# One core's attention and experts kernel: the first expert's last 640 tokens in Strassen's form, the attention blocks packed closer

## The chip, the core and the metric

One core of one Trainium2 chip. The metric is device time in microseconds (us), of the whole program. TensorE is PE in the profile, VectorE DVE, ScalarE ACT, GpSimd POOL, SyncE SP; L757 is line 757 of the kernel before.

## The reference

All in fp32: attention in a band, then four experts, then one layer with a rational function.

```
scores = q k^T / 8, masked to a band (4 plain heads: the last 32 keys; 4 dilated: every 4th of 128)
x   = softmax(scores) v                    -> 1152 tokens x 512
for e in 0..3: x2 += p[:, e] * (relu(x @ w1[e]) @ w2[e])       w1 512x1024, w2 1024x512
h   = x2 @ w_in;  g = P(h) / (Q(h) + 1e-6);  out = g @ w_out   w_in 512x2048
```

## The kernel before

**Precision.** Every operand of TensorE is split in a high and a low part (fp32r): ScalarE copies the high part, VectorE or GpSimd subtracts for the low one, and each product is three matmuls: hi hi, hi lo, lo hi.

**Iterations.** `ITER` lists (expert, first token, tokens). Expert 0 has four, of 256, 256, 256 and 384 tokens; experts 1 to 3 have two each, of 640 and 512; then six of 384 for the rational layer, which is kept as two more experts. An iteration has 8 chunks (`FC`) of 128 hidden columns. Slot (k, f): `inner_product(k, f)` makes a chunk of h (4 x 3 matmuls, L673), ScalarE takes relu of it (`high`), VectorE the low part (`low`), and `outer_product` of the chunk `LAG` = 3 slots before adds h w2 into the sums of each tile of 128 tokens (3 matmuls of 512 columns for each tile, L757). `take_sums` (VectorE) keeps the sums.

**Strassen's form** (in Winograd's variant, L731) is used by experts 1 to 3: chunks go in 4 pairs, each pair in 7 products of half the tokens and half the depth (6 matmuls each) in place of 8. It needs sums of weight quarters S1 to S4 (`sum_pair` on GpSimd, `high_pair` on ScalarE, `low_pair` on GpSimd) and of token quarters T1 to T4 (`transform` on VectorE, `high_t` on ScalarE, `low_t` on VectorE), and `combine` on VectorE makes the quarters C of the result by way of U2 and U3. `snapshot` (ScalarE) copies "A11 B11" out before "A12 B21" is added to it. The T parts of tokens 0 to 640 and 640 to 1152 are made beside the 384-token iteration of expert 0 and serve all three experts.

**Attention** comes in 20 blocks of two heads: 16 big ones (256 tokens: units 0 to 3 times 4 head pairs) and 4 small ones (the 128 tokens that remain). A block w goes: `scores(w)` on TensorE; `mask`, `maximum` on VectorE; `exponentials` on ScalarE (4 of big, 2 of small); `invert` on VectorE; `normalise` on GpSimd; `turn(w)` on TensorE; `take_turned` on ScalarE; `values(w)` on TensorE; `attention_hi` on ScalarE, `attention_lo` on VectorE. In a slot with block w TensorE does inner product, `turn(w)`, outer product, `values(w)`, `scores(w + 2)`, and the helpers do the softmax of w + 1. Blocks 0 to 5 come in a part written out by hand ahead of slot (0, 4). `block_of_slot` puts blocks 6 to 19 in every second slot of iterations 0 and 1, in slot (1, 7), and in slots 0 to 6 of iteration 2; the 384-token iteration has none.

**Order.** Each engine runs one written list, and waits only by semaphores; nothing overtakes. GpSimd's list holds `normalise(w)`, the low parts of expert 0's weights (`low_w1`, `low_w2`) and the mask of the small dilated blocks (`make_rest_mask`, a string of selects). SyncE issues all loads in one list (`load_qk`, `load_v`, `load_inner`, `load_outer`, `load_raw1`); a load waits until its buffer is read.

```
            normalise(9)
            make_rest_mask()
            for w in range(10, BLOCKS):
                normalise(w)
```

## Time and profile before

| | us |
|---|---|
| runs | 641.30, 641.62, 642.65: median 641.62 |
| profiled execution | 640.78, its span 639.0 |
| TensorE busy | 631.6 |
| VectorE, ScalarE, GpSimd busy | 389.6, 318.0, 269.1 |
| L757 outer products, chain's share | 46% |
| L673 plain inner products, chain's share | 23% |
| L731 Strassen products, chain's share | 20% |

The span is the time from the first instruction to the last. Matmuls overlap, so a matmul's own duration is longer than its distance to the next; the chain of waits shows the distance. The granted clock of TensorE is full in all 40 slices of the span.

### The profile page before, as it was taken

How to read it: one execution, taken by the hardware profiler on the slowest of the kernel's cores; microseconds unless marked ns; L12 is line 12 of the kernel's file. 1: busy time of each engine (PE TensorE's matmuls, PEld its weight loads, DVE VectorE, ACT ScalarE, POOL GpSimd, SP SyncE). 2: the span in 40 equal slices, each digit the busy share in tenths (PEclk: the TensorE clock that was granted, in tenths of full speed). 3: DMA queues.
4: the chain of work that ended last, by engine and by line, in shares of the span. 5: the costliest groups of instructions: out<-in, count | busy, mean ns of one | idle time of the engine just before them, and what ended most of it. 6: DMA issues, size and time to landing. Idle time of an engine off the chain costs nothing.

```text
span 639.0 us, 10664 instructions
## 1 busy us (share of the span) xinstructions
PE 631.6 (99%) x4008; PEld 561.5 (88%) x4008; DVE 389.6 (61%) x760; ACT 318.0 (50%) x740; POOL 269.1 (42%) x283
## 2 busy tenths in 40 slices
PE   8999999999999999999999999999999999999998
PEld 6888888898888898898899898889998999889996
DVE  6534543937755445325456325438988788889896
ACT  6864552335322333212343212346887777877774
POOL 6763112049830794301784101145712576732221
PEclk9999999999999999999999999999999999999999
DMA  8942210002220131000122100101530000001011
GB/s 289 292 157 87 72 34 1 2 33 73 94 66 2 67 100 66 34 2 2 66 100 67 34 0 2 67 34 52 186 126 1 1 1 1 2 0 50 2 49 51
DMA packets 21684, 37.68 MB, mean 59 GB/s; under 512 B 3520, under 2 KB 4160, under 8 KB 21632
## 3 DMA queue, kind: packets, MB, share of 16 engines
q1 hardware_dynamic: 21632, 36.99, 17.5%
q8 instruction: 32, 0.52, 0.3%
q14 instruction: 20, 0.16, 0.1%
HBM read 34.62 MB, written 2.36 MB: 58 GB/s over the span
## 4 chain that ended last, share of the span: by engine, by line
PE 93%; SPq 2%; DVE 2%; ACT 1%; DMA 1%; issue 1%; POOL 0%; DVEq 0%; ACTq 0%
PE banks L757 46%; PE banks L673 23%; PE banks L731 20%; PE banks L645 1%; PE banks L616 1%; PE banks L626 1%; DMA scratch<-in_qk_dil 1%; ACT scratch L881 1%; SPq L562 1%; PE banks L793 1%; PE banks L633 0%; SPq L507 0%; DVE h_lo L1300 0%; DVE acc L1206 0%; DVE acc L1201 0%
## 5 line engine op out<-in xcount | busy, mean ns | idle before, releaser
L757 PE MATMUL banks<-w_hi,h_hi 128*128 128x512 f32 x432 | 171.7, 397 | 0.1
L757 PE MATMUL banks<-w_lo,h_hi 128*128 128x512 f32 x432 | 170.6, 395 | 0.0
L757 PE MATMUL banks<-w_hi,h_lo 128*128 128x512 f32 x429 | 169.9, 396 | 0.0
L1520 POOL TENSOR_TENSOR w_lo<-raw,w_hi 128x512 fp32r<-128x512 f32 x32 | 41.2, 1310 | 157.8 <-ACT w_hi L934 157.8
L673 PE MATMUL banks<-x_hi,w_hi 128*128 128x384 f32 (+1 forms) x320 | 104.9, 328 | 0.0
L673 PE MATMUL banks<-x_lo,w_hi 128*128 128x384 f32 (+1 forms) x320 | 102.5, 320 | 0.0
L673 PE MATMUL banks<-x_hi,w_lo 128*128 128x384 f32 (+1 forms) x320 | 102.3, 320 | 0.0
L1293 DVE TENSOR_TENSOR stage<-banks,stage 128x320 f32<-128x320 f32 (+1 forms) x120 | 54.1, 455 | 78.1 <-PE banks L731 74.9
L757 PEld LDWEIGHTS banks<-w_hi,h_lo 128*128 128x128 f32 x429 | 80.5, 188 | 19.3
L757 PEld LDWEIGHTS banks<-w_lo,h_hi 128*128 128x128 f32 x432 | 81.2, 188 | 14.5
L757 PEld LDWEIGHTS banks<-w_hi,h_hi 128*128 128x128 f32 x432 | 81.2, 188 | 14.6 <-issue 0.4
L1534 POOL TENSOR_TENSOR h_lo<-rational,h_hi 128x384 fp32r<-128x384 f32 x47 | 47.7, 1015 | 108.6 <-ACT h_hi L1092 108.6
L979 ACT ACTIVATE h_hi<-stage 128x320 fp32r<-128x320 f32 (+1 forms) x72 | 31.4, 443 | 79.6 <-DVE stage L1293 79.4
L1300 DVE SCALAR_TENSOR_TENSOR h_lo<-stage,h_hi 128x320 fp32r<-128x320 f32 (+1 forms) x72 | 54.6, 768 | 24.6 <-ACT h_hi L979 23.2
L1493 POOL TENSOR_TENSOR w_lo<-raw,w_hi 128x512 fp32r<-128x512 f32 x40 | 53.8, 1359 | 28.9 <-ACT w_hi L917 28.3
L673 PEld LDWEIGHTS banks<-x_hi,w_hi 128*128 128x128 f32 x320 | 60.2, 188 | 4.6 <-DVE rational L1391 0.2
L673 PEld LDWEIGHTS banks<-x_lo,w_hi 128*128 128x128 f32 x320 | 60.3, 188 | 2.4
L673 PEld LDWEIGHTS banks<-x_hi,w_lo 128*128 128x128 f32 x320 | 60.3, 188 | 0.0
L1066 ACT ACTIVATE banks<-banks,b_sb 128x384 f32<-128x384 f32 x48 | 26.7, 556 | 36.4 <-PE banks L673 36.3
L1386 DVE SCALAR_TENSOR_TENSOR rational<-rational,b_abs,banks 128x384 f32<-128x384 f32 x48 | 29.4, 613 | 23.5 <-ACT rational L1067 23.2
L962 ACT ACTIVATE stage<-banks 128x320 f32<-128x320 f32 (+1 forms) x24 | 9.9, 410 | 58.0 <-PE banks L731 57.8
L1467 POOL TENSOR_TENSOR scratch<-scratch 128x384 f32<-128x384 f32 (+1 forms) x20 | 15.4, 772 | 50.3 <-DVE scratch L1164 50.2
(119 smaller groups left out, 1238.0 us busy)
## 6 DMA issues: line engine op xcount, KB each, us to landing
raw<-in_weights SPq DMA_DIRECT2D x48, 256.0 KB, 2.9
raw<-in_weights SPq DMA_DIRECT2D x16, 512.0 KB, 3.6
raw_last<-in_weights SPq DMA_DIRECT2D x16, 256.0 KB, 5.9
scratch<-in_v SPq DMA_DIRECT2D x16, 192.0 KB, 4.9
scratch<-in_qk_dil SPq DMA_DIRECT2D x8, 320.0 KB, 5.5
out_t<-acc SPq DMA_DIRECT2D x9, 256.0 KB, 2.1
scratch<-in_qk_plain SPq DMA_DIRECT2D x8, 272.0 KB, 4.4
scratch<-in_qk_rest SPq DMA_DIRECT2D x2, 256.0 KB, 2.8
```

Source lines behind the costliest of these rows:

```text
L673: last = nc.tensor.matmul(h_of(k, f), w[:, f, dc, :], x, start=dc == 0 and i == 0, stop=dc == DC - 1 and i == 2)
L731: last = nc.tensor.matmul(product_bank(name)[:, 0:n], w[:, d], x[:, d], start=opens and d == 0 and i == 0, stop=d == HALF - 1 and i == 2, ...
L757: last = nc.tensor.matmul(sum_bank(k, t), h[:, cols], w[:, f, :], start=f == 0 and i == 0, stop=f == FC - 1 and i == 2)
L979: nc.scalar.activation(quarter(k, p, name)[0], source, ACT.Relu).then_inc(quarter_hi, 1)
L1066: nc.scalar.activation(ps_q[:, 0:WIDE], h_of(k, f), ACT.Abs, scale=b_sb[:, 0:1])
L1293: nc.vector.tensor_tensor(out, bank, to, ALU.add).then_inc(combined, 1)
L1300: nc.vector.scalar_tensor_tensor(out=lo, in0=source[:, 0:n], scalar=0.0, in1=hi.bitcast(F32), op0=ALU.max, op1=ALU.subtract).then_inc(quar ...
L1386: nc.vector.scalar_tensor_tensor(out=qq[:, i], in0=sq[:, i], scalar=b1_abs[:, 0:1], in1=ps_q[:, 0:WIDE], op0=ALU.mult, op1=ALU.add).then_i ...
L1467: nc.gpsimd.tensor_tensor(p, p, row_inv[:, w % SOFT, 0:n].unsqueeze(2).to_broadcast([P, n, TK]), ALU.mult).then_inc(normed, 1)
L1493: nc.gpsimd.tensor_tensor(w2_lo[:, c], raw_of(e, c)[1], w2_hi[:, c].bitcast(F32), ALU.subtract)\
L1520: last = nc.gpsimd.tensor_tensor(w1_lo[:, 2 * p + c].rearrange("p a b -> p (a b)"), raw1[:, c], w1_hi[:, 2 * p + c].rearrange("p a b -> p ...
L1534: nc.gpsimd.tensor_tensor(h3_lo[:, c % RING, :], h_full[:, c % SLOTS], h3_hi[:, c % RING, :].bitcast(F32), ALU.subtract)\
```

## The change

- Expert 0 has three iterations: two of 256 tokens (tokens 640 to 896 and 896 to 1152) and, as iteration `KW` = 2, one of 640 tokens (0 to 640) in Strassen's form. Units are laid in token order so that units 0 and 1 are the first two iterations (`UNIT_AT`).
- Blocks 8 to 19 are reordered (`SEQUENCE`), head pairs 0 and 2 first. `VISITS` gives every slot from (0, 3) to (1, 6) a block, and (1, 1) and (1, 6) two. TensorE's turn(6) follows scores(7) with no product between. Outer products of a slot with two blocks go one tile to each block.
- T parts of tokens 0 to 640 are made beside slots (1, 2) to (1, 5) and (1, 7), those of the rest beside iteration 3. ScalarE copies them behind each slot's block steps.
- S parts of expert 0 are made by GpSimd between the normalises, and high_pair by ScalarE in slots (1, 2), (1, 4), (1, 7) and the first pair of iteration 2. Expert 0's raw weight pairs are loaded once more (`load_raw1(0, p)`).
- GpSimd's `make_rest_mask` moves behind normalise(10), low_w2(5) ahead of it. ScalarE's copies of expert 0's weights spread over more slots.
- The first Strassen pair has its own order of products, with two outer products between the first ones.
- On-chip memory is laid out anew (offsets only), and load order follows the blocks.

The diff, cut to what matters here; SyncE's list first, then TensorE, ScalarE, VectorE, GpSimd:

```diff
 FILLERS = (6, 2, 3, 2, 1)
-MASK_AT = (0, PAIRS // 2, BIG_BLOCKS)
+SEQUENCE = [(u, p) for u in (0, 1) for p in range(PAIRS)]
+SEQUENCE += [(u, p) for d in (0, 1) for u in range(2, UNITS + 1) for p in (d, d + PAIRS // 2)]
+VISITS = {(0, 3): (6,), (0, 4): (7,), (0, 5): (8,), (0, 6): (9,), (0, 7): (10,),
+          (1, 0): (11,), (1, 1): (12, 13), (1, 2): (14,), (1, 3): (15,), (1, 4): (16,), (1, 5): (17,), (1, 6): (18, 19)}
+MASK_AT = (0, PAIRS // 2, SEQUENCE.index((UNITS, 0)))
...
 WIDE = 3 * P
-ITER = [(0, 0, 2 * P), (0, 2 * P, 2 * P), (0, 4 * P, 2 * P), (0, 6 * P, WIDE)]
+ITER = [(0, 5 * P, 2 * P), (0, 7 * P, 2 * P), (0, 0, 5 * P)]
...
+KW = START[1] - 1
+PLAIN_CHUNKS = KW * FC
+UNIT_AT = (5 * P, 7 * P, 0, 2 * P, 4 * P)
...
-W1_HIGH_AT = ((4,), (), (5, 6), (), (7,), (), (), ())
-W2_HIGH_AT = ((0, 1), (), (2,), (), (3,), (4,), (5,), (6, 7))
+W1_HIGH_AT = ((4,), (), (5,), (6,), (7,), (), (), ())
+W2_HIGH_AT = ((0,), (), (1,), (2,), (3,), (4,), (5,), (6, 7))
...
-T_STEPS = (((0, 0, 0), (0, 0, 1)), ((0, 1, 0),), ((0, 1, 1),), ((1, 0, 0), (1, 0, 1)), ((1, 1, 0),), ((1, 1, 1),), (), ())
+T_STEPS = {2: ((0, 0),), 3: ((0, 1),), 4: ((0, 2),), 5: ((0, 3),), FC - 1: ((1, 0), (1, 1), (1, 2))}
+T_STEPS_MIDDLE = {2: ((0, 3),), 3: ((1, 2),)}
+T_STEPS_END = {0: ((0, 0),), 1: ((0, 1), (0, 2)), 2: ((1, 0), (1, 1)), 3: ((1, 3),)}
+T_OF_STEP = (("T1",), ("T3", "T2"), ("T4",), ())
+S_HIGH_AT = {2: 0, 4: 1, FC - 1: 2}
...
+            load_v(10)
+            load_qk(12)
+            for w in range(11, 15):
+                load_v(w)
+                load_qk(w + 2)
+            load_raw1(0, 0)
+            for w in range(15, 18):
+                load_v(w)
+                load_qk(w + 2)
+            load_v(18)
+            load_raw1(0, 1)
+            load_v(19)
             sp.dma_start(a_sb[:, :], a.partition_broadcast(P)).then_inc(ab_in, 16)
             sp.dma_start(b_sb[:, :], b.partition_broadcast(P)).then_inc(ab_in, 16)
-            for w in range(2 * PAIRS, 3 * PAIRS):
-                load_qk(w)
-                load_v(w)
+            load_raw1(0, 2)
+            load_raw1(0, 3)
             load_raw1(1, 0)
             for c in (0, 1):
                 load_raw2(1, c)
-            for w in range(3 * PAIRS, BLOCKS):
...
-                    w = block_of_slot(k, f)
-                    inner_product(k, f)
-                    if w is not None:
+                    ws = visits(k, f)
+                    if (k, f) != (0, LAG):
+                        inner_product(k, f)
+                    if not ws:
+                        outer_of_slot(k, f)
+                    for i, w in enumerate(ws):
                         turn(w)
-                    outer_of_slot(k, f)
-                    if w is not None:
+                        outer_of_slot(k, f, range(i, i + 1) if len(ws) > 1 else None)
                         values(w)
                         if w + 2 < BLOCKS:
                             scores(w + 2)
-            for f in range(FC):
-                inner_product(UNITS - 1, f)
-                outer_of_slot(UNITS - 1, f)
-            outer_product(UNITS - 1, FC - LAG)
-            for k in range(START[1], START[MOE]):
+            outer_product(KW - 1, FC - LAG)
+            winograd_product(KW, 0, "A11 B11")
+            outer_of_pair(KW, 0, 0)
+            winograd_product(KW, 0, "A12 B21")
+            outer_of_pair(KW, 0, 1)
+            for name in FIRST_PRODUCTS[2:]:
+                winograd_product(KW, 0, name)
+            for k in range(KW, START[MOE]):
                 for p in range(FP):
...
-                        continue
-                    high(k, f)
-                    if w is not None:
-                        take_turned(w)
-                        if k == 0 and f < LAG:
-                            high(k, f + 1)
-                        if w + 1 < BLOCKS:
-                            exponentials(w + 1)
-                        attention_hi(w)
+                    if (k, f) == (0, 2):
+                        high(0, 2)
+                        take_turned(5)
+                        high(0, 3)
+                        exponentials(6)
+                        attention_hi(5)
+                    elif k or f > LAG:
+                        high(k, f)
+                    for w in visits(k, f):
+                        steps_of_block(w)
                     if k == 0:
                         for c in W1_HIGH_AT[f]:
                             high_w1(c)
                         for c in W2_HIGH_AT[f]:
                             high_w2(0, c)
+                    else:
+                        for d, step in T_STEPS.get(f, ()):
+                            high_t_of_step(0, d, step)
+                        if f in S_HIGH_AT:
+                            high_pair(0, S_HIGH_AT[f])
             act.wait_ge(ab_in, 32)
             nc.scalar.activation(b1_abs[:, :], b_sb[:, 1:2], ACT.Abs).then_inc(b1_ready, 1)
-            for f in range(FC):
-                high(UNITS - 1, f)
-                for g, d, half in T_STEPS[f]:
-                    for t in ("T4",) if half else ("T1", "T3", "T2"):
-                        if (g, t) != (1, "T1"):
...
+                if step == 0:
+                    dve.wait_ge(xa_lo, BLOCKS if g or d else BLOCKS - PAIRS - 2)
...
-                    if w is not None and w + 1 < BLOCKS:
-                        mask(w + 1)
-                    if w is not None and w > PAIRS:
+                    ws = visits(k, f)
+                    for i, w in enumerate(ws):
+                        if w + 1 < BLOCKS:
+                            mask(w + 1)
                         attention_lo(w - 1)
-                    if w is not None and w + 1 < BLOCKS:
-                        maximum(w + 1)
-                    low(k, f)
-                    if k == 1 and f == 0:
+                        if w + 1 < BLOCKS:
+                            maximum(w + 1)
+                        if i == 0 and (k, f) != (0, LAG):
+                            low(k, f)
+                        if w + 1 < BLOCKS:
+                            invert(w + 1)
+                    if not ws:
+                        attention_lo(BLOCKS - 1)
+                        low(k, f)
+                    if (k, f) == (1, 0):
                         normalise_probs()
-                    if k == 0 and f < LAG:
-                        low(k, f + 1)
-                    if w is not None and w + 1 < BLOCKS:
-                        invert(w + 1)
                     if k and f == LAG - 1:
                         take_sums(k - 1)
-                    if w == BLOCKS - 1:
-                        attention_lo(w)
-            for f in range(FC):
-                if f == LAG - 1:
-                    take_sums(UNITS - 2)
-                low(UNITS - 1, f)
-                for g, d, half in T_STEPS[f]:
-                    transform(g, d, half)
-            for k in range(START[1], START[MOE]):
+                    if k:
+                        for d, step in T_STEPS.get(f, ()):
+                            transform(0, d, step)
+            transform(0, 1, 3)
+            for k in range(KW, START[MOE]):
...
             normalise(6)
             low_w1(0, 5)
+            low_w2(0, 1)
+            normalise(7)
+            low_w1(0, 6)
             low_w2(0, 2)
-            low_w1(0, 6)
-            normalise(7)
+            normalise(8)
+            low_w1(0, 7)
             low_w2(0, 3)
-            low_w1(0, 7)
+            normalise(9)
             low_w2(0, 4)
-            normalise(8)
             low_w2(0, 5)
+            normalise(10)
+            make_rest_mask()
             low_w2(0, 6)
+            normalise(11)
             low_w2(0, 7)
             nc.gpsimd.memset(log_bias[:, :], ONE_EPS * 2.0 ** -LOG_SHIFT)
             nc.gpsimd.memset(exp_bias[:, :], -LOG_SHIFT * math.log(2.0))
-            normalise(9)
-            make_rest_mask()
-            for w in range(10, BLOCKS):
-                normalise(w)
+            normalise(12)
+            normalise(13)
+            sum_pair(0, 0)
+            normalise(14)
+            normalise(15)
+            low_pair(0, 0)
+            normalise(16)
+            sum_pair(0, 1)
+            normalise(17)
+            low_pair(0, 1)
+            normalise(18)
+            normalise(19)
+            for p in (2, 3):
+                sum_pair(0, p)
+                low_pair(0, p)
```

## Rows read from the trace of the kernel before

**Rows 1.** The page, part 1: engine, busy us (share of span), instructions.
```profile
PE 631.6 (99%) x4008; PEld 561.5 (88%) x4008; DVE 389.6 (61%) x760; ACT 318.0 (50%) x740; POOL 269.1 (42%) x283
```

**Rows 2.** Waits of PE: who waited for whom: us in total, times, longest.
```profile
PE banks L731 <- DVE stage L1293: 0.9, 1, 0.9
```

**Rows 3.** The chain, 0 to 260 us: start us, us, what.
```profile
35.29 1.43 PE banks L673 x12
...
69.21 1.62 PE banks L673 x12
70.83 0.44 PE banks L626 x4
71.27 1.40 PE banks L757 x6
72.67 0.61 PE banks L645 x16
73.28 0.49 PE banks L616 x16
...
82.42 0.33 PE banks L616 x16
...
88.78 0.22 PE banks L626 x2
...
105.76 2.09 PE banks L673 x12
...
164.38 4.40 PE banks L731 x30
```

**Rows 4.** PE in order of time, about 26 us: start us, us, engine, line, what.
```profile
25.52 0.56 PE L616 MATMUL banks<-scratch 64*64 64x96 f32 x16
```

**Rows 5.** ACT in order of time, 70 to 135 us.
```profile
71.31 0.59 ACT L891 ACTIVATE scratch<-banks 96x512 f32<-96x512 f32 x1
...
73.33 0.63 ACT L895 ACTIVATE x_hi<-banks 128x256 fp32r<-128x256 f32 x1
...
133.33 0.83 ACT L937 ACTIVATE s_hi<-s_stage 128x768 fp32r<-128x768 f32 x1
```

**Rows 6.** POOL in order of time, 26 to 140 us.
```profile
27.24 0.83 POOL L1467 TENSOR_TENSOR scratch<-scratch 128x384 f32<-128x384 f32 x1
...
43.55 1.28 POOL L1493 TENSOR_TENSOR w_lo<-raw,w_hi 128x512 fp32r<-128x512 f32 x1
...
47.92 1.02 POOL L1436 TENSOR_SCALAR_AFFINE_SELECT scratch<-scratch 32x96 f32<-32x96 f32 x3
49.20 4.84 POOL L1436 TENSOR_SCALAR_AFFINE_SELECT scratch<-scratch 32x48 f32<-32x48 f32 x13 [0.26 <-POOL scratch L1436]
...
73.81 0.83 POOL L1467 TENSOR_TENSOR scratch<-scratch 128x384 f32<-128x384 f32 x1 [3.74 <-DVE scratch L1164]
...
86.62 0.51 POOL L1467 TENSOR_TENSOR scratch<-scratch 128x192 f32<-128x192 f32 x1 [2.85 <-DVE scratch L1164]
...
105.86 0.73 POOL L1513 TENSOR_TENSOR raw<-raw 128x256 f32<-128x256 f32 x1
...
135.50 1.85 POOL L1526 TENSOR_TENSOR s_lo<-s_stage,s_hi 128x768 fp32r<-128x768 f32 x1
```

**Rows 7.** DVE in order of time, 86 to 115 us.
```profile
86.46 1.39 DVE L1201 TENSOR_SCALAR acc<-banks,prob 128x512 f32<-128x512 f32 x2
...
108.89 0.88 DVE L1218 TENSOR_TENSOR stage<-x_hi,x_lo 128x320 f32<-128x320 f32 x2
109.81 0.49 DVE L1241 TENSOR_TENSOR stage<-stage 128x320 f32<-128x320 f32 x1
...
113.12 1.29 DVE L1226 TENSOR_TENSOR t_lo<-stage,t_hi 128x320 fp32r<-128x320 f32 x3
```

**Rows 8.** Line L1300 between 139 and 168 us: duration ns min/median/max.
```profile
L1300 DVE SCALAR_TENSOR_TENSOR h_lo<-stage,h_hi x6: 543/1498/2105, 146.9 to 162.0; 128x320 fp32r<-128x320 f32 x6
L1300 DVE SCALAR_TENSOR_TENSOR h_lo<-banks,h_hi x2: 476/484/492, 143.7 to 154.3; 128x320 fp32r<-128x320 f32 x2
```

More of the change, by code:

```diff
@@ L74 @@
 PRODUCTS = ("A11 B11", "S2 T2", "S1 T1", "A12 B21", "S3 T3", "A22 T4", "S4 B22")
+FIRST_PRODUCTS = ("A11 B11", "A12 B21", "S2 T2", "S1 T1", "S3 T3", "A22 T4", "S4 B22")
 COMBINED = ("U2", "U3", "C22", "C21", "C12")
@@ L486, in load_qk @@
             def load_qk(w):
-                pair, n = w % PAIRS, qk_columns(w)
+                slot, pair, n = w % PAIRS, pair_of(w), qk_columns(w)
                 if w >= PAIRS:
@@ L603, in scores @@
             def scores(w):
[L605 to L606 removed]
+                slot, rows, first_key = w % PAIRS, tile_rows(w), tokens_of_block(w)
+                pe.wait_ge(qk_in[slot], 16 * (w // PAIRS + 1))
                 if w >= 2:
@@ L613, in scores @@
                     for half in (0, 1):
-                        buf = qk[half * HD:(half + 1) * HD, pair, :]
+                        buf = qk[half * HD:(half + 1) * HD, slot, :]
                         key = first_key + t * key_step(w)
@@ L635, in values @@
             def values(w):
-                pair, rows = w % PAIRS, tile_rows(w)
+                slot, rows = w % PAIRS, tile_rows(w)
                 pe.wait_ge(pt_ready, w + 1)
-                pe.wait_ge(v_in[pair], 16 * (w // PAIRS + 1))
+                pe.wait_ge(v_in[slot], 16 * (w // PAIRS + 1))
                 if w >= 2:
@@ L645, in values @@
                         last = nc.tensor.matmul(value_bank(w)[half * HD:(half + 1) * HD, t * rows:(t + 1) * rows],
-                                                vv[0:TK, pair, half, t, :], pt[0:TK, w % 2, col:col + rows],
+                                                vv[0:TK, slot, half, t, :], pt[0:TK, w % 2, col:col + rows],
                                                 start=True, stop=True)
@@ L749, in outer_product @@
                 hi, lo = h_parts(k, f)
-                for t in range(tiles_of(k)):
+                for t in part:
                     if f == 0 and k:
@@ L953, in snapshot, with high_t_of_step @@
+            def high_t_of_step(g, d, step):
+                for t in T_OF_STEP[step]:
+                    high_t(g, d, t)
             def snapshot(k, p):
@@ L1055, in _ @@
                             high_w2(e + 1, c)
+                    if k == START[1]:
+                        for d, step in T_STEPS_END.get(p, ()):
+                            high_t_of_step(1, d, step)
                     if x2[1:]:
@@ L1330, in _ @@
             high_w1(3)
-            for k in range(UNITS - 1):
+            mask(5)
+            maximum(5)
+            low(0, 0)
+            low(0, 1)
+            invert(5)
+            mask(6)
+            attention_lo(4)
+            maximum(6)
+            low(0, 2)
+            low(0, 3)
+            invert(6)
+            for k in range(KW):
                 for f in range(FC):
-                    w = block_of_slot(k, f)
-                    if k == 0 and f in (1, 3):
+                    if k == 0 and f < LAG:
@@ L1360, in _ @@
+            transform(0, 1, 3)
+            for k in range(KW, START[MOE]):
                 for p in range(FP):
@@ L1370, in _ @@
                         low_x2(x2[0])
+                    if k == START[1]:
+                        for d, step in T_STEPS_MIDDLE.get(p, ()):
+                            transform(1, d, step)
                     combine(k, p, "C21")
@@ L1376, in _ @@
                         low_x2(x2[1])
-                    if k == START[1] and p in (2, 3):
-                        low_t(1, p - 2, "T1", t1_stage[:, p - 2, :])
-                    if k == START[1] and p in (1, 2):
-                        transform_t1(p - 1)
+                    if k == START[1]:
+                        for d, step in T_STEPS_END.get(p, ()):
+                            transform(1, d, step)
             def from_h(k, f):
```

315 lines of the change are left out of this document (160 added, 155 removed).

## The prediction

> **What bounds the kernel now.** I read the page's head first, then who waited for whom, then the chain that ended last, slot by slot, and then each helper engine's order of work beside it. A slot (k, f) is chunk f of iteration k: an inner product, the outer product of three chunks before, and, where an attention block is packed in, its turn (transposes), values and the scores of the block two further on. TensorE is busy all but a few microseconds of the span [rows 1]; its one wait past the start is 0.9 us, for a VectorE sum at the first Strassen pairs [rows 2]. So time is saved only by taking work off TensorE, and a helper that comes late costs its whole lateness.
>
> A slot with a big block is 1.62 + 0.44 + 1.40 + 0.61 + 0.49 = 4.56 us, and 4.40 where the scores are those of a small block (0.33) [rows 3]. One slot in two carries a block in iterations 0 and 1 now, that is one per 7.4 us; only iteration 2 has one in each. Beside a block runs a loop of the helpers: ScalarE takes the turned block at 71.31 and its four exponentials end by 73.33, VectorE inverts, GpSimd normalises from 73.81 for 0.83, and the next turn can start at 74.7 [rows 5, 6]. From turn to turn the loop needs 3.85 us if nothing else stands in it. The slot gives 4.56: 0.7 us to spare.
>
> **What it removes.** Iterations 2 (256 tokens) and 3 (384) become one of 640 in Strassen's form. Out go 8 inner products of 1.62 and 8 of 2.10: 29.8 us. In come 4 x 7 x 6 = 168 products, 4.40 us for 30 [rows 3]: 24.6. The inner products that follow another outer product now take 1.43; six of them get a block before them and become 1.62: 1.1 back. The outer products are the same in number and size. Gain 4.05 us, and the 0.9 us wait is recosted below: 4.95.
>
> **What it adds: waits of TensorE, by its own timetable.** Times are the profile's clock until they part.
>
> First, block 6. Its turn now follows scores(7) at once, with no inner product or outer product ahead. TensorE is free at 26.08 [rows 4]; GpSimd normalises block 6 from 27.24 to 28.07 [rows 6], tied to block 6's exponentials, which stand behind the same inner product (0, 3) in both kernels. Wait 2.05.
>
> Second, low_w2(5) stands ahead of normalise(10) on GpSimd, but its copy high_w2(5) is now the last thing ScalarE does in slot (0, 6), after block 9's values. The copy (about 0.55, as another copy of 512 columns) and the split, 1.28 [rows 6], come after the exponentials in place of an idle 0.6 us: normalise(10) ends about 0.95 us after TensorE wants turn(10). Wait 0.95, between 0 and 1.3.
>
> Third, and largest, make_rest_mask. It is a string of 16 selects, each waiting for the last, and fills GpSimd from 47.92 to 54.18 [rows 6]. Today it lies in a 7.4 us gap and just fits. Now it stands between normalise(10) and normalise(11), with low_w2(6) behind it: 6.26 + 1.28 + 0.83 = 8.35 us from one normalise's end to the next's, where TensorE has one slot of 4.40. Wait 3.95, between 3.5 and 4.4.
>
> Fourth, two blocks in a slot, (1, 1) and (1, 6). Between their turns TensorE has 0.22 + 0.70 (one tile of outer products) + 0.59 + 0.49 = 2.0 us; the small loop takes, from the first turn's start, 0.22 + 0.30 + 0.72 (two exponentials) + 0.57 + 0.51 [rows 6] = 2.3. Wait 0.35 in (1, 1). Behind it GpSimd has sum_pair(0, 0), four sums ending with the one at 105.86, 3.07 us in all [rows 6], ahead of normalise(14): turn(14) comes 0.65 late. In (1, 6) VectorE also has the last three splits of a T column, 1.29 [rows 7], ahead of mask(19): 1.5.
>
> Fifth, the T parts. ScalarE's copies of T stand in each slot behind attention_hi, and ahead of the next slot's high and take_turned. In (1, 2) VectorE ends invert(15), then keeps iteration 0's sums, 1.39, then sums for 1.41 (from 108.89 to 110.30) before T1 is there [rows 7]. ScalarE stands still for it, copies T1 (0.4), and then has high_pair(0, 0), 0.3 + 0.74 [rows 5]; take_turned(15) ends 1.55 us after TensorE wants values(15). In (1, 3), T3 and T2 give 0.45. In (1, 4), T4 with high_pair(0, 1) gives 1.7. Sum 3.7, between 1 and 5.5. The queue is what costs here: 0.5 us copies that wait 2 to 3 us for VectorE hold up the whole loop.
>
> So attention gains 2.05 + 0.95 + 3.95 + 0.35 + 0.65 + 1.5 + 3.7 = 13.15 us of waits.
>
> Sixth, the first Strassen pair. Transform (0, 1) can start only when slot (1, 7)'s split is done, 2.45 us into it, and its last copy ends 4.8 us later; high_pair(0, 2) follows (1.05), and only then comes snapshot(2, 0), on which "A12 B21" waits: 8.7 us into the slot, where TensorE is there after 1.62 + 1.40 + 1.40 + 0.88 + 1.40 = 6.7. Wait 2.0. Then five products run with no outer product between: "A22 T4" waits for U3, 0.55. high_pair(0, 3), between the copies of C11 and C22, waits for a sum of GpSimd's that waits for a load and for low_pair(0, 2); C22, C21 and with it the next pair's "S2 T2" come 2.2 late, if the split of C22 meets low_pair's 1.85 us instruction [rows 6]. U2 of that pair stands behind two tiles of sums (0.9 now, with three): 0.5. Sum 5.25, between 1.5 and 8.
>
> Seventh, iteration 3's pair 1 is the place of today's 0.9 us wait, behind three tiles of sums. Now there are five (1.4 more) and a T step (1.41): 2.0, between 0 and 3.7.
>
> Port: the split of a quarter out of the staging buffer took 0.54 to 2.1 us, median 1.5, in the stretch where GpSimd was busy; out of a bank it took 0.48 [rows 8]. I have put one such collision into the sixth term and none into the fifth. The Trainium skill (SBUF — State Buffer, "two separate sides") calls this an exclusive lock held for a whole instruction, between GpSimd and VectorE instructions with two SBUF inputs. The trace agrees. By that rule T's sums, which have both inputs in SBUF and today run with GpSimd idle, would each wait for a GpSimd instruction of 0.8 to 1.85 us, and the fifth term would go to its upper bound.
>
> Costed at nothing: the loads. Block 8's load, issued at 26.58 today, goes out near 16.6, others later; a load is 0.44 us of issue and about 5 us to land, and each is issued over a slot ahead. If that cover goes, each load costs its lateness, up to 2 us. Memory laid out anew costs nothing in itself.
>
> **Sum.** 640.78 (this execution; span 639.0) - 4.95 + 13.15 + 5.25 + 2.0 = 656.2. The median of the runs lies 0.84 above this execution: 657.0.
>
> **Rivals.** (A) The forecast, 657: every helper wait counts. For it: 0.7 us to spare in the loop. Against it: my fifth to seventh terms rest on ScalarE's and VectorE's order worked through.
>
> (B) ScalarE's T copies and the first Strassen pairs hold nothing up; only the first four terms count (9.45) and the 0.9 stays: 640.78 - 4.05 + 9.45 + 0.84 = 647.0. For it: values has 1.40 us of outer product ahead of it as cover. Against: T1 is behind 2.8 us of VectorE work.
>
> (C) The clock. Granted clock is full in every stretch of this profile, also over the short waits at the start, so nothing here shows a fall. If the nearly 4 us wait of TensorE at turn(11) brings the clock from 2.4 to 1.2 GHz, the slot after it takes up to twice its 4.56 us: up to 4.6 us on top, part of it cover for the helpers. 660, up to 662. The Trainium skill (TensorE: Matmul & The Clock Gate, "HAM oscillation") says that idle TensorE is taken to half its clock; no run here shows it yet.
>
> (D) The other side: TensorE stays the bound. It is decided at one place, the mask's string of selects: if it runs beside the slots without normalise(11) being late, the packed loop as a whole has room, the other waits shrink with it, and only the work counts: 641.62 - 4.95 = 636.7. For it: iteration 2 today runs a block in each slot with no wait. Against: it needs 8.35 us of GpSimd's work within 4.40 us, or more than 4 us of slack that the loop doesn't have. The kernel is no slower only if all waits together stay under 4.95 us; the first three alone are 6.95.
>
> **Chances.** A 0.62, B 0.15, C 0.15, D 0.05, no visible change 0.03. The likeliest gives 657.0. A's bounds are 651 to 664; to hold B as well the range goes down to 647, and up to 663 with C. A difference below 0.2% (1.3 us) can't be told from none here. Faster 0.05, within 0.2% 0.03, slower 0.92.
>
> **What would show it.** After: TensorE's busy share near 96%; a wait of 3.5 to 4.4 us of a transpose for GpSimd's normalise about 30 us after block 6's; one of 2 us near 26; four or five of 0.4 to 2 us for ScalarE's take_turned, or of values; 2 us at "A12 B21" for the snapshot. Some 168 more Strassen matmuls and 192 fewer plain ones. The forecast is wrong if the mask's stretch shows no wait, if ScalarE's T copies show no idle time ahead of them while values run on time, or if the granted clock falls.

## The result, and the profile after

| | before | after |
|---|---|---|
| median of the runs, us | 642.13 (641.30 to 642.91, 4 runs) | 661.84 (659.58 to 664.65, 4 runs) |
| ratio, 95% interval | | 1.0309 [1.0264, 1.0354] |
| profiled execution, its span | 640.78, 639.0 | 664.65, 662.6 |
| mean granted clock | 1.0 in the profile | 0.987, 0.992, 0.995, 0.992 |

The change costs 19.7 us; 15.4 were predicted over the 641.62 shown. The profiled execution of after is the slowest of its four runs, and the one with the lowest clock: its times below carry some 3 us more of that loss than the median does.

The page of the kernel after, parts 1 and 2 (the engine's busy time and its share; then 40 equal slices), beside [rows 1]:

```profile
PE 638.4 (96%) x3984; PEld 564.1 (85%) x3984; DVE 396.3 (60%) x774; ACT 324.3 (49%) x752; POOL 290.7 (44%) x307
...
PEclk9997998999999999999999999999999999999999
```

Two things are to be seen. TensorE has 24 instructions fewer and is busy 6.8 us *longer* than in [rows 1]; and the fourth and the seventh slice (50 to 66 and 99 to 116 us) show why: the granted clock isn't full any more. The 4008 - 3984 = 24 matmuls are the 168 added and 192 taken out.

Waits of TensorE in after, whole span (who waited for whom: us in total, times, longest), where [rows 2] stood:

```profile
PE banks L679 <- POOL scratch L1539: 9.7, 7, 4.0
PE banks L698 <- ACT scratch L953: 3.1, 3, 1.5
PE banks L785 <- ACT stage L1025: 2.8, 2, 2.0
PE banks L785 <- DVE stage L1354: 2.6, 4, 1.5
```

L679 is `turn` waiting for normalise, L698 `values` waiting for take_turned, L785 the Strassen products waiting for a snapshot (L1025) or for VectorE's sums (L1354). Each is shown in time by its first instruction after the wait (TensorE in order of time in after, 15 to 191 us: start, length, engine, line, what, and in brackets the idle time before and who ended it):

```profile
29.23 0.64 PE L679 MATMUL banks<-ident,scratch 128*96 128x128 f32 x4 [2.07 <-POOL scratch L1539]
...
50.18 0.64 PE L679 MATMUL banks<-ident,scratch 128*96 128x128 f32 x4 [1.04 <-POOL scratch L1539]
...
54.51 0.28 PE L726 MATMUL banks<-x_hi,w_lo 128*128 128x256 f32 x1
58.79 1.09 PE L679 MATMUL banks<-ident,scratch 128*96 128x128 f32 x4 [4.00 <-POOL scratch L1539]
...
81.91 0.69 PE L698 MATMUL banks<-scratch 96*64 96x64 f32 x16 [1.47 <-ACT scratch L953]
...
93.58 0.69 PE L698 MATMUL banks<-scratch 96*64 96x64 f32 x16 [1.12 <-ACT scratch L953]
...
98.89 0.42 PE L679 MATMUL banks<-ident,scratch 128*96 128x128 f32 x2 [1.16 <-POOL scratch L1539]
...
109.16 0.63 PE L785 MATMUL banks<-x_hi,w_hi 128*128 128x320 f32 x1 [2.04 <-ACT stage L1025]
...
177.11 0.41 PE L785 MATMUL banks<-t_hi,w_hi 128*128 128x320 f32 x1 [1.50 <-DVE stage L1354]
```

These are turn(6), turn(10), turn(11) (the row at 54.51 is the last product ahead of it), values(15), values(17), turn(19), "A12 B21" and iteration 3's pair 1. Behind turn(11)'s wait of 4.00 stands what was predicted (GpSimd in after, in order of time): normalise(10) at 49.30, the 16 selects, low_w2(6), and only then normalise(11) at 57.90.

```profile
49.30 0.82 POOL L1539 TENSOR_TENSOR scratch<-scratch 128x384 f32<-128x384 f32 x1
50.08 1.37 POOL L1508 TENSOR_SCALAR_AFFINE_SELECT scratch<-scratch 32x96 f32<-32x96 f32 x4
51.96 4.48 POOL L1508 TENSOR_SCALAR_AFFINE_SELECT scratch<-scratch 32x96 f32<-32x96 f32 x12 [0.51 <-POOL scratch L1508]
56.50 0.09 POOL L1533 MEMSET scratch<- 1x1 f32 x1
56.67 1.27 POOL L1565 TENSOR_TENSOR w_lo<-raw,w_hi 128x512 fp32r<-128x512 f32 x1
57.90 0.84 POOL L1539 TENSOR_TENSOR scratch<-scratch 128x384 f32<-128x384 f32 x1
```

**Where all of it went.** The whole difference lies ahead of iteration 4, whose first product (256 columns) starts at 190.52 in before and at 214.10 in after: 23.6 us, and the spans differ by 23.6. From inner product (0, 0) to there, by the windows view (from:to, length, TensorE busy, granted clock), first before, then after:

```profile
15.53:190.52 174.99, 173.57 (x1382) 1.00 0.27 84
```

```profile
16.15:214.10 197.95, 179.51 (x1357) 0.96 0.27 85
```

Idle time goes from 1.4 to 18.4 us: 17.0 more. Busy time goes up by 5.9 instead of down by 4.05; what the clock has in that is seen where a kernel with the same matmuls ran at full clock in this stretch (e9_more below): 171.14. So the work itself is 2.4 us less, and the clock costs 179.51 - 171.14 = 8.4 us in this execution. (Two more kernels with the same matmuls in nearly the same order, e6_orders and e11_best, have 171.60 and 171.72 there at full clock: by them the work is 1.9 us less and the clock costs 7.8 to 7.9.) -2.4 + 17.0 + 8.4 = 23.0, and 0.6 is a later start (15.53 to 16.15), which also varies between profiles of one kernel.

**The clock.** It falls at the long waits. TensorE and its clock in after (same view; behind the busy time stand the number of matmuls, then the granted clock, 1.00 for 2.4 GHz and 0.50 for 1.2):

```profile
52.00:56.00 4.00, 2.79 (x45) 1.00 0.50 164
56.00:60.00 4.00, 1.21 (x5) 0.74 0.29 105
60.00:64.00 4.00, 4.00 (x31) 0.50 0.00 0
64.00:68.00 4.00, 4.00 (x20) 0.50 0.36 119
68.00:72.00 4.00, 4.00 (x67) 0.98 0.39 115
```

The clock fell near 58 us, some 0.8 us before turn(11)'s wait ended at 58.79, and until about 68 us TensorE ran at 1.2 GHz. Its matmuls show it: one of an outer product takes 0.63 us in place of 0.39 to 0.41. In sum (length of a stretch times what its clock lacks of full) 30 to 35, 55 to 70 and 105 to 115 us lose 8.6 us, and 662.6 x (1 - 0.987) is 8.6 too. By the same product the runs with a clock of 0.992 lose 5.3 us and the one with 0.995 loses 3.3. Less these amounts the four runs of after lie 1.9 us apart, where as measured they lie 5.1 apart.

### The profile page after: what moved, and what is told of

It reads as the page before. It is cut to its first block, busy times and chain, and to the rows that moved or that the text cites. A ratio compares the mean times of both kernels' runs of the same rounds, so it can differ in the third digit from the quotient of the medians.

```text
span 662.6 us, 10696 instructions
## 1 busy us (share of the span) xinstructions
PE 638.4 (96%) x3984; PEld 564.1 (85%) x3984; DVE 396.3 (60%) x774; ACT 324.3 (49%) x752; POOL 290.7 (44%) x307
## 4 chain that ended last, share of the span: by engine, by line
PE 84%; DVE 6%; ACT 3%; issue 3%; POOL 2%; DMA 1%; SPq 1%; POOLq 0%; ACTq 0%; DVEq 0%
PE banks L813 42%; PE banks L785 22%; PE banks L726 17%; ACT scratch L943 2%; DMA raw<-in_weights 1%; POOL scratch L1539 1%; PE banks L679 1%; DVE acc L1272 1%; PE banks L698 1%; POOL scratch L1508 1%; PE banks L849 1%; DVE stage L1354 1%; PE banks L669 0%; DVE s_stage L1289 0%; POOL w_lo L1565 0%
## 5 line engine op out<-in xcount | busy, mean ns | idle before, releaser
L813 PE MATMUL banks<-w_hi,h 128*128 128x512 f32 x512 | 169.8, 395 | 0.0
L1354 DVE TENSOR_TENSOR stage<-banks,stage 128x320 f32<-128x320 f32 (+1 forms) x140 | 64.0, 461 | 101.6 <-PE banks L785 97.4
L813 PEld LDWEIGHTS banks<-w_hi,h 128*128 128x128 f32 x512 | 96.1, 188 | 20.6
L813 PE MATMUL banks<-w_lo,h 128*128 128x512 f32 x256 | 101.2, 395 | 0.0
L1042 ACT ACTIVATE h<-stage 128x320 fp32r<-128x320 f32 (+1 forms) x84 | 37.0, 447 | 99.1 <-DVE stage L1354 98.8
L726 PE MATMUL banks<-x_hi,w_lo 128*128 128x384 f32 (+1 forms) x256 | 83.0, 324 | 0.0
L1361 DVE SCALAR_TENSOR_TENSOR h<-stage,h 128x320 fp32r<-128x320 f32 (+1 forms) x84 | 54.9, 661 | 25.4 <-ACT h L1042 23.1
L813 PE MATMUL banks<-w_lo,h_hi 128*128 128x512 f32 x144 | 56.7, 394 | 0.0
L813 PE MATMUL banks<-w_hi,h_hi 128*128 128x512 f32 x144 | 56.7, 394 | 0.0
L813 PEld LDWEIGHTS banks<-w_lo,h 128*128 128x128 f32 x256 | 48.1, 188 | 9.4
L813 PE MATMUL banks<-w_hi,h_lo 128*128 128x512 f32 x141 | 56.0, 397 | 0.0
L1025 ACT ACTIVATE stage<-banks 128x320 f32<-128x320 f32 (+1 forms) x28 | 11.5, 412 | 54.3 <-PE banks L785 53.8
```

Source lines behind the costliest of these rows:

```text
L726: last = nc.tensor.matmul(h_of(k, f), w[:, f, dc, :], x, start=dc == 0 and i == 0, stop=dc == DC - 1 and i == 2)
L813: last = nc.tensor.matmul(sum_bank(k, t), h[:, cols], w[:, f, :], start=f == 0 and i == 0, stop=f == FC - 1 and i == 2)
L1042: nc.scalar.activation(quarter(k, p, name)[0], source, ACT.Relu).then_inc(quarter_hi, 1)
L1354: nc.vector.tensor_tensor(out, bank, to, ALU.add).then_inc(combined, 1)
L1361: nc.vector.scalar_tensor_tensor(out=lo, in0=source[:, 0:n], scalar=0.0, in1=hi.bitcast(F32), op0=ALU.max, op1=ALU.subtract).then_inc(quar ...
```

## The experiments

Ratios are to the kernel before on the same chip (medians 641.5 to 642.0).

### e1_fill: the clock alone

Matmuls whose result isn't used fill part of three waits, so the waits are as long but TensorE isn't idle in them.

```diff
+FILL_AT = {6: 5, 11: 11}
...
+                        fill(turned_bank(w), FILL_AT.get(w, 0))
                         turn(w)
...
             outer_of_pair(KW, 0, 0)
+            for _ in range(7):
+                nc.tensor.matmul(ps_b, w1_hi[:, 0, 0, :], x_hi[:, 0, 0:512], start=True, stop=True)
             winograd_product(KW, 0, "A12 B21")
```

> The changed kernel with TensorE kept at work in its three longest waits: 5 spare products before turn(6), 11 before turn(11) (0.25 us each), 7 of 512 columns before 'A12 B21'. The waits stay as long as they are. If the lowered clock costs time (the changed profile has 17 us at 1.2 GHz, mostly over work), the granted clock becomes 1.00 in the stretches 30 to 35, 55 to 70 and 105 to 115 us and the time falls by 5 to 9 us, to 653 to 657, and the runs lie closer together. If the clock is not what makes the rest of the difference, the time stays within 1.5 us of 661.8.

Measured: 658.74 us (658.02 to 661.06, 5 runs), ratio 1.0277 [1.0260, 1.0294]; clocks 1.0, 1.0, 0.999, 0.997, 0.991. So work was added, and the kernel became faster: by 2.1 us by the ratios, 3.1 by the medians (the intervals overlap). The idle time that is left ahead of turn(11) is 1.5 us, and the engine is at full speed behind it:

```profile
56.52 0.64 PE L680 MATMUL banks<-ident,scratch 128*96 128x128 f32 x4 [1.54 <-POOL scratch L1543]
...
57.24 0.39 PE L814 MATMUL banks<-w_lo,h_parts_plain 128*128 128x512 f32 x1
```

A full clock is worth 2 to 3 us of the median, under the 5 to 9 expected. The reason is in the same profile: a slow TensorE gives late helpers time. TensorE now waits 1.76 us for a Strassen sum that was 0.26 late in after, where the slow products ahead of it had covered it (TensorE in e1_fill):

```profile
113.21 0.41 PE L786 MATMUL banks<-t_hi,s_hi 128*128 128x320 f32 x1 [1.76 <-DVE stage L1358]
```

From inner product (0, 0) to iteration 4 e1_fill takes 191.90 us, 20.8 over the 171.14 of work without fillers: waits and fillers together are 2.3 us more than after's 18.4 of waits. The clock's 5.3 us of a typical run, less these 2.3, are the 3 measured.

### e5_mask: the string of selects cut in three

`make_rest_mask` does 4 selects ahead of normalise(5), 8 ahead of low_w2(5) and 4 behind normalise(10).

```diff
+            make_rest_mask(0, 4, (w1_lo_done, 4))
             normalise(5)
...
+            make_rest_mask(4, 12, (w2_lo_done, 5))
             low_w2(0, 5)
             normalise(10)
-            make_rest_mask()
+            make_rest_mask(12, 16, (normed, 11))
             low_w2(0, 6)
```

> The changed kernel with make_rest_mask cut in three: 4 selects behind low_w1(3), 8 behind low_w2(4), 4 behind normalise(10). If the string of selects is what turn(11) waits 4.0 us for, that wait goes, and with it the clock's fall behind it (some 2 of the 3 us that the kept clock gave): 654.5 to 657. If other work of the packed loop takes the mask's place (low_w2(6), the exponentials), 2 us or more of wait stay before turn(11), and the time is above 658.

Measured: 657.55 us (656.89 to 658.47, 4 runs), ratio 1.0243 [1.0228, 1.0258]: 4.3 us less than after, a little less than expected. TensorE in order of time:

```profile
48.33 0.64 PE L679 MATMUL banks<-ident,scratch 128*96 128x128 f32 x4 [1.55 <-POOL scratch L1546]
...
54.31 0.64 PE L679 MATMUL banks<-ident,scratch 128*96 128x128 f32 x4 [1.36 <-POOL scratch L1546]
```

The 4.00 us wait is 1.36 now, but turn(10)'s went from 1.04 to 1.55 (eight selects stand ahead of its normalise), and the wait for the Strassen sum is 1.83. Idle time in the stretch fell only by 2.1 us (18.4 to 190.90 - 174.53 = 16.4), busy time by 5.0. That 5.0 is what the clock had cost behind turn(11)'s wait alone, half speed from 58 to 68 us: e5_mask's own clock fell twice, like after's at its two waits of 2 us, but elsewhere, 1.8 us after values(15)'s wait of 1.47 us had ended and 1.6 us after that of the Strassen sum (TensorE and its clock in e5_mask, windows view):

```profile
75.00:80.00 5.00, 5.00 (x36) 0.66 0.19 55
110.00:115.00 5.00, 3.91 (x19) 0.77 0.60 200
```

On the medians, too, the 4.3 us are about half idle time and half clock (0.992 in after's middle runs, 0.995 in e5_mask's: 2 us). Beside normalise(11) there are still four selects and low_w2(6), where it should be one of the two.

### e7_before_mask: the same string in the kernel before

To see whether the string costs its length only where the loop is full, it was moved in the kernel *before* into iteration 2, which has a block in each slot.

```diff
-            normalise(9)
-            make_rest_mask()
-            for w in range(10, BLOCKS):
+            for w in range(9, BLOCKS):
                 normalise(w)
+                if w == 14:
+                    make_rest_mask()
```

> The kernel before with one thing changed: make_rest_mask stands between normalise(14) and normalise(15), where slots are 4.57 us, in place of behind normalise(9), where they are 7.4. Mask and normalise take 7.1 us from 74.64, turn(15) wants them at 79.97: a wait of 1.8 us, time 1.5 to 2.0 us up, to 643.1 to 643.6, and more only if the clock falls. If a late normalise is absorbed by work ahead on TensorE, the time stays within 0.5 us of 641.5.

Measured: 644.06 us (643.52 to 644.81, 6 runs), ratio 1.0033 [1.0021, 1.0045]. Waits of TensorE in this kernel:

```profile
PE banks L626 <- POOL scratch L1467: 2.7, 4, 1.9
```

One new wait of 1.9 us (1.8 was worked out), and 2.1 us on the median, just over what was expected. The clock explains the rest: three of the six runs have a granted clock of 1.0 (643.52, 643.60, 643.80: at or just over the upper bound expected), three of 0.997 (644.31, 644.76, 644.81). The profiled one is of those; its matmuls of an outer product take 0.63 us just behind the wait:

```profile
87.65 0.63 PE L757 MATMUL banks<-w_lo,h_hi 128*128 128x512 f32 x1
```

Where the same string stood in before it costs nothing [rows 6]. Its price is its length less the room around it, nothing of its own.

### e3_tcopies and e8_tmid: why the T copies are late

Two ways to help the fifth term. e3_tcopies leaves VectorE's order and lets ScalarE copy each T part a slot later:

```diff
-T_STEPS = {2: ((0, 0),), 3: ((0, 1),), 4: ((0, 2),), 5: ((0, 3),), FC - 1: ((1, 0), (1, 1), (1, 2))}
+T_STEPS = {2: ((0, 0),), 3: ((0, 1),), 4: ((0, 2),), 6: ((0, 3),), FC - 1: ((1, 0), (1, 1), (1, 2))}
+T_COPIES = {3: ((0, 0),), 4: ((0, 1),), 5: ((0, 2),), FC - 1: ((1, 0), (1, 1), (1, 2))}
```

> ScalarE's T copies one slot later, VectorE's last splits of the first T column in slot (1, 6) in place of (1, 5). VectorE's work is the same. If ScalarE's standing still ahead of T copies is the cause, the three waits for take_turned (1.47, 0.51, 1.12 us) fall to 0.3 each or less: 2.3 us or more faster, 659.5 or less. If it is VectorE's amount of work (mask(w + 1) late behind sums and T steps), they turn into waits of turns for normalise of about the same length and less than 1 us is gained.

Measured: 662.35 us (660.15 to 663.68, 4 runs), ratio 1.0322 [1.0299, 1.0344]: no gain. ScalarE isn't held up by its copies any more, but VectorE then is late itself. VectorE's two sums for T1 in e3_tcopies, then in after:

```profile
77.09 2.78 DVE L1290 TENSOR_TENSOR stage<-x_hi,x_lo 128x320 f32<-128x320 f32 x2
```

```profile
78.16 0.88 DVE L1289 TENSOR_TENSOR stage<-x_hi,x_lo 128x320 f32<-128x320 f32 x2
```

The two sums took 2.78 us instead of 0.88, while GpSimd was in this instruction (e3_tcopies again):

```profile
77.44 2.08 POOL L1606 TENSOR_TENSOR s_lo<-s_stage,s_hi 128x768 fp32r<-128x768 f32 x1
```

The Trainium skill (SBUF — State Buffer, "two separate sides") says that a VectorE instruction with two SBUF inputs and a GpSimd instruction that reads SBUF shut each other out, each for its whole length. The trace agrees: the second sum alone lasted 2.12 us, until just behind the end of GpSimd's 2.08. GpSimd was in that instruction so early because ScalarE, with no T1 to wait for, had made high_pair(0, 0) sooner. Behind the sums, mask and maximum and the exponentials were late, and `values` waited 2.15 us, up to 81.52, for `attention_lo`. So ScalarE's copies alone aren't it: where T's sums stand in VectorE's list, and what GpSimd does meanwhile, counts too.

e8_tmid changes where they stand: in slots (1, 3) to (1, 6), a slot later than in after, VectorE makes them between `low` and `invert`, where it would otherwise stand still for the exponentials. ScalarE's copies come a slot later with them, still behind its block steps.

```diff
+T_STEPS = {3: ((0, 0),), 4: ((0, 1),), 5: ((0, 2),), 6: ((0, 3),), FC - 1: ((1, 0), (1, 1), (1, 2))}
...
                             low(k, f)
+                        if k and i == 0:
+                            for d, step in T_STEPS.get(f, ()):
+                                transform(0, d, step)
                         if w + 1 < BLOCKS:
                             invert(w + 1)
```

> The changed kernel with VectorE's T steps moved from behind invert to the gap between low and invert, one slot later; ScalarE's copies stay behind attention_hi, in the same slot, where T is now ready. If both ScalarE's standing still and VectorE's late masks come from where the T steps stand, the three waits (1.47, 0.51, 1.12 us) fall to under 0.9 in all: 659 to 660. If it is the shared work (GpSimd's pairs against VectorE's two-input sums), T steps of twice the length push invert late and turns wait for normalise by 0.5 to 1.5 in these slots: no gain, 661 to 663.

Measured: 659.58 us (657.81 to 662.18, 4 runs), ratio 1.0277 [1.0254, 1.0300]. No wait of L698 for ScalarE's L953 is left (3.1 us in after), and idle time in the stretch is 3.4 us less (18.4 to 192.58 - 177.58 = 15.0). The median is 2.3 us lower, but its interval overlaps after's; the idle time is what shows the gain. The fifth term was an order, not an amount of work; whether the place in the list or the slot's delay did it, this run doesn't separate.

### e10_strassen: the order around the first pairs

snapshot(2, 0) ahead of T4's copy, high_pair(0, 3) behind C12's copy, and the T steps of iteration 3 spread evenly.

```diff
-T_STEPS_MIDDLE = {2: ((0, 3),), 3: ((1, 2),)}
-T_STEPS_END = {0: ((0, 0),), 1: ((0, 1), (0, 2)), 2: ((1, 0), (1, 1)), 3: ((1, 3),)}
+T_STEPS_MIDDLE = {1: ((0, 0),), 2: ((0, 2),), 3: ((1, 1),)}
+T_STEPS_END = {1: ((0, 1),), 2: ((0, 3), (1, 0)), 3: ((1, 2), (1, 3))}
...
+                            if (d, step) == (1, 2):
+                                snapshot(KW, 0)
                             high_t_of_step(0, d, step)
```

> The changed kernel with only the order around the Strassen pairs of expert 0 mended: snapshot(2, 0) ahead of the copy of T4, high_pair(0, 3) behind the copy of C12, and the T steps of tokens 640 to 1152 spread evenly over iteration 3. The attention part is untouched, so its 12.5 us of waits stay. Theory (each wait of the trace costs its own length, whatever stands around it): of the 3.12 us at the first pair 0.8 stay (U3 0.6, and 0.2), and the 2.2 us of iteration 3 go, so 4.5 us less than the changed kernel: 657.3, and 656.5 if the fall of the clock at 105 to 115 us goes with the 2.0 us wait. Rival (the helpers are late as a whole by then, and a step moved out of one place costs in the next): under 2 us less, 660 or more.

Measured: 655.50 us (652.79 to 656.87, 5 runs), ratio 1.0205 [1.0180, 1.0230]: 6.3 us less than after. Of the 5.3 us of waits 1.4 are left, 0.6 more than worked out, and iteration 3 has none; idle time in the stretch is 3.9 us less (18.4 to 188.14 - 173.62 = 14.5). The rest is the clock: it fell only behind turn(11)'s wait in this profile, not at 30 and not at 105 us.

```profile
PE banks L785 <- ACT stage L1025: 0.8, 1, 0.8
PE banks L785 <- DVE stage L1357: 0.6, 1, 0.6
```

### e6_orders: all orders mended

e5_mask, e8_tmid and e10_strassen together, low_w2(5) and low_w2(6) behind the normalise of their slot, sum_pair(0, 0) behind normalise(14), and slot (0, 3)'s outer product ahead of turn(6). No work is added or left out.

```diff
+            normalise(10)
             low_w2(0, 5)
-            normalise(10)
-            make_rest_mask()
+            make_rest_mask(12, 16, (w2_lo_done, 6))
+            normalise(11)
             low_w2(0, 6)
-            normalise(11)
...
+            normalise(14)
             sum_pair(0, 0)
-            normalise(14)
...
+                    if (k, f) == (0, LAG):
+                        outer_of_slot(k, f)
                     for i, w in enumerate(ws):
                         turn(w)
```

> All orders mended at once: mask cut up, low_w2(5) behind normalise(10), an outer product ahead of turn(6), sum_pair(0, 0) behind normalise(14), VectorE's T steps in the gap between low and invert, snapshot(2, 0) ahead of T4's copy, high_pair(0, 3) behind C12, iteration 3's T steps behind U2. If the order of the helpers' lists is all that makes the change slow, what is left is the Strassen gain less some 2 us of small waits: 638 to 642. If the packed loop can't be kept within the slot whatever the order, waits of 0.5 us or more stay in most slots and the time is above 645.

Measured: 643.59 us (642.04 to 644.48, 12 runs), ratio 1.0022 [1.0012, 1.0032], over the 638 to 642 expected and under the rival's 645. turn(6)'s wait is 0.42 with 0.68 at values(6), turn(10)'s 0.32, and turn(11) and iteration 3 don't wait; turn(19)'s is still 1.14. By the ratios 0.0287 of the 0.0309 are gone, 18 of the 20 us, and the kernel is still no faster than before, though it was to have 4 us less work.

### e9_more and e11_best: is there a version that beats both?

e9_more moves one T step out of the slot with two blocks, and the first pair's second outer product to where TensorE waited for U3:

```diff
+                    if (k, f) == (1, FC - 2):
+                        transform(0, 0, 3)
...
             winograd_product(KW, 0, "A12 B21")
+            for name in FIRST_PRODUCTS[2:5]:
+                winograd_product(KW, 0, name)
             outer_of_pair(KW, 0, 1)
-            for name in FIRST_PRODUCTS[2:]:
+            for name in FIRST_PRODUCTS[5:]:
```

> The kernel with all orders mended, and two more: the T step (0, 3) behind both blocks of slot (1, 6), and the second outer product of the first Strassen pair moved to between "S3 T3" and "A22 T4". Theory: turn(19)'s wait of 1.14 us falls to about 0.1 to 0.4 and the 0.58 us for U3 goes, 1.3 us in all: 642.3, with the fastest runs at 641, that is no difference from the kernel before that can be told. What is then left over against its 3.1 us less TensorE work (4.05 by the prediction's count) are waits of 0.2 to 0.7 us, some 2.5 together. Rival (the step moved comes late for T4's low part at the first pair, or the products now without an outer product between wait for their banks): no gain over 643.6.

Measured: 642.84 us (641.66 to 644.10, 11 runs), ratio 1.0014 [1.0005, 1.0023], which can't be told from e6_orders. The U3 wait is gone and turn(19)'s is 0.86, but the second pair's snapshot is 1.38 late, behind high_pair(0, 3). The windows view of e9_more over the same work, at full clock:

```profile
16.15:192.53 176.38, 171.14 (x1358) 1.00 0.32 96
```

171.14 against 173.57 before: the reorganised kernel has 2.4 us less for TensorE to do (1.9 by the 171.60 and 171.72 of e6_orders and e11_best), not 4.05, and 5.2 us of idle time against 1.4.

e11_best takes away the wait that e9_more had made:

```diff
                         snapshot(k, p)
+                    if (k, p) == (KW, 1):
+                        high_pair(0, FP - 1)
...
                     high_quarter(k, p, "C12")
-                    if k == KW and p == 0:
-                        high_pair(0, FP - 1)
```

> e9_more with high_pair(0, 3) moved from behind the copy of C12 of the first pair to behind snapshot(2, 1), since in e9_more ScalarE stood still for GpSimd's sum_pair(0, 3) there and "A12 B21" of the second pair waited 1.38 us for the snapshot behind it. Theory (that one wait hangs on that one place in ScalarE's list): the 1.38 us go, 641.4 to 641.6, 0.0 to 0.5 us under the kernel before and not to be told from it. Rival (GpSimd is late as a whole there, so low_pair(0, 3) or the sums of the next expert make the next wait): 642.5 or more, as e9_more.

Measured: 643.60 us (642.39 to 644.66, 12 runs), ratio 1.0015 [0.9995, 1.0035]. The rival held: the wait moved again, to where it said, the sums of the next expert. GpSimd's first of them waits 2.75 us for its load, ScalarE stands 7.46 us for the last with the copies of C22 and C21 behind it, and VectorE's sum comes late. GpSimd, ScalarE and TensorE in e11_best:

```profile
107.42 0.73 POOL L1599 TENSOR_TENSOR s_stage<-raw 128x256 f32<-128x256 f32 x1 [2.75 <-DMA raw<-in_weights]
...
110.52 1.15 ACT L1004 ACTIVATE w_hi<-raw 128x512 fp32r<-128x512 f32 x2 [7.46 <-POOL raw L1605]
...
114.59 0.41 PE L785 MATMUL banks<-t_hi,s_hi 128*128 128x320 f32 x1 [1.05 <-DVE stage L1362]
```

No version here beats the kernel before. By these numbers the most that is to be had is the 1.9 to 2.4 us, if every wait but before's own goes. That was not reached, and whether it can be stays open. No run tried to get the raw weights in earlier.

## Why the prediction held, point by point

The time (657, range 647 to 663) was right in sign and range and 4.8 us low. The median from the parts: 642.13 - 2.4 + 17.0 + 5.3 (clock at 0.992) = 662.0, against 661.84. So the direction and the waits were foreseen, but 661.84 is nearer to rival C's 660 to 662 (chance 0.15) than to A's 657, and it came no further out because waits that were over-sized made up in part for a gain that was over-counted and a clock that was left out. One of the prediction's own signs of being wrong, a fall of the granted clock, came true as well.

| Term | predicted | after | where |
|---|---|---|---|
| Strassen's form, TensorE's work | -4.05 | -2.4 | windows |
| 1 turn(6) | 2.05 | 2.07 | 29.23 |
| 2 turn(10) | 0.95 | 1.04 | 50.18 |
| 3 turn(11), mask | 3.95 | 4.00 | 58.79 |
| 4 two blocks, sum_pair | 2.5 | 1.84 | 0, 0.68, 1.16 |
| 5 T copies | 3.7 | 3.52 | 1.47, 0.51, 0.42, 1.12 |
| 6 first pair | 5.25 | 3.12 | 2.04, 0.58, 0.26, 0.24 |
| 7 iteration 3 | 2.0 | 2.22 | 1.50, and 0.72 for a snapshot that wasn't named |
| clock | 0 (rival C: up to 4.6) | 5.3 (8.4 in the profile) | windows |

**The waits** held, in most terms to 0.2 us, and where an experiment took a cause away the wait shrank or went: e5_mask took 2.6 of the third term's 4.0, e8_tmid the waits of the fifth for ScalarE, e10_strassen 3.9 of the 5.3 of sixth and seventh. The causes of the first and second were taken away only in e6_orders, with all the others. Rival B (T copies and first pair hold nothing up) and D (TensorE stays the bound) fell with them.

**The sixth term** looks over-sized at 3.12 against 5.25. At full clock it was nearer: e5_mask, where the clock was full over the first products, has 2.04 + 0.58 + 1.83 = 4.45. In after TensorE ran at 1.2 GHz just behind the snapshot's wait, and the C21 that was to be 2.2 late was only 0.26 late. In the fourth, too, turn(13) waits 0.43 in e5_mask, e8_tmid and e10_strassen and not at all in after, where the slot was slowed.

**What failed first: the gain.** The step "six of them get a block before them and become 1.62: 1.1 back" under-counted. Counted in the traces from each matmul's start to the next one's, without waits, the 16 plain inner products that stay take 26.1 us in e9_more. In before all 32 take 53.5, and the 16 that go are 29.3 of them (29.8 in the prediction); that leaves 24.2 for the 16. So 1.9 come back instead of 1.1. From slot (0, 4) on, every second one took 1.42 to 1.44 us in before and the others 1.53; in e9_more all take 1.53 to 1.69. The turns cost 0.6 more as well (4.9 to 5.4). The Strassen products were right: 24.5 against 24.6.

**What failed second: the clock at nothing.** Before showed full clock over its short waits, and the prediction took that for the forecast, with the fall as a rival at 0.15 and only behind turn(11). The mechanism of the rival happened: in after, e3_tcopies, e8_tmid and e10_strassen the granted clock was at half from within the wait of 4.0 us on, for 7 to 10 us. It also fell behind both waits of 2 us in after and e8_tmid, and behind turn(6)'s in e3_tcopies, which rival C had not counted. The Trainium skill (TensorE: Matmul & The Clock Gate, "HAM oscillation"), by which a TensorE left idle goes to half its clock, was weighed as a rival there; the trace agrees with it at the wait of 4.0 us (0.50 in the windows 60:64 and 64:68). The two misses, 1.6 and about 5, less the 2.5 by which the waits came out under the forecast, are most of the 4.8.

**Loads** were costed at nothing. TensorE itself waits for none after inner product (0, 0); ahead of it a wait of 0.8 us stands where before had one of 0.7. But GpSimd's sum_pair(0, 3) waits 1.94 us for its raw weights in after and 2.03 in e5_mask, and through high_pair(0, 3) that is in the late C22 of the sixth term, as the prediction's words there say. How much of that term the load makes was not measured. GpSimd in e5_mask:

```profile
104.17 0.73 POOL L1586 TENSOR_TENSOR s_stage<-raw 128x256 f32<-128x256 f32 x1 [2.03 <-DMA raw<-in_weights]
```

## What to carry to other kernels

When helpers run in a closed loop with the bound engine, write down the loop's slack for each slot before packing it tighter; every step that is moved in costs its length less that slack, wherever it comes from, and here most such waits could be worked out beforehand to a few tenths of a microsecond. Price a long wait of TensorE (here 1.5 us and more) at more than its length, since the work behind it may run at half clock; and don't add up waits measured under a fallen clock, because slow work ahead hides the next one. Before counting a gain in work, price what stays by the neighbours it will have, not by those it had.

## What the runs showed of the hardware that was not expected

- The clock doesn't fall after each wait of the same length. Behind turn(6)'s wait of 2.07 us the matmuls went to 0.63 us in after, and with 2.06 us in e5_mask they stayed at 0.39 to 0.41. In order of time, after and then e5_mask:

```profile
30.18 0.68 PE L813 MATMUL banks<-w_hi,h_parts_plain 128*128 128x512 f32 x2
30.65 0.63 PE L813 MATMUL banks<-w_lo,h_parts_plain 128*128 128x512 f32 x1
```

```profile
29.28 0.62 PE L813 MATMUL banks<-w_hi,h_parts_plain 128*128 128x512 f32 x2
29.74 0.40 PE L813 MATMUL banks<-w_lo,h_parts_plain 128*128 128x512 f32 x1
```

- Shorter waits were followed by a fall too: one of 1.90 us in e7_before_mask, and ones of 1.83 and 1.47 us in e5_mask. The wait of 1.47 at values(15) stands in after and e10_strassen as well, and there the clock stayed full behind it.
- Kernels with such waits scatter more: after's four runs lie 5.1 us apart with clocks from 0.987 to 0.995, the slowest with the lowest; e5_mask's four (0.992 to 0.997) and before's first four lie 1.6 apart.
- One wait of 4 us costs twice: behind turn(11)'s the clock stood at half from about 58 to 68 us in after, which is 5.2 of the 8.6 us that the clock took there. In e8_tmid and e10_strassen it stood so for 7 us behind the same wait.
- Two VectorE sums with both inputs in SBUF took 2.78 us beside GpSimd, the second of them 2.12 beside one instruction of 2.08, and 0.88 together without it. An instruction of GpSimd can so hold up a chain that doesn't wait for GpSimd in the program at all.
